# High and low planes in one stationary operand, four projections per head instead of six

## The reference

```python
q_bits = (np.einsum('bhsd,dk->bhsk', q, proj) > 0)      # 6 bits, same for k
mask = q_bucket[:, :, :, None] == k_bucket[:, :, None, :]
scores = np.where(mask, scale * q @ k.T, -1e9)
attn = softmax(scores)                                   # sum + 1e-9
x = attn @ v                                             # 2 batches, 8 heads, 768 positions, 64 wide
x = elu(x @ w_in) @ w_out                                # 1536 tokens, 512 -> 2048 -> 512
out = (s * relu(x @ w2_in)**2 + b) @ w2_out
```

## Time and profile before

| | us |
|---|---|
| median of 3 runs | 739.97 (739.96 to 742.11) |
| profiled execution | 740.75 |
| its span, first to last instruction | 738.9 |
| PE busy | 729.4 (99%) |
| DVE busy | 558.3 (76%) |
| ACT busy | 502.0 (68%) |
| POOL busy | 497.3 (67%) |

### The profile page before, as it was taken

The page is one execution under the profiler, slowest core; times in us unless marked ns, Lnnn a source line. Parts: engine busy times, 40 slices in busy tenths (PEclk is TensorE's granted clock), DMA queues, the critical chain, the costliest instruction groups (busy, mean ns, idle before and its releaser), DMA issues.

```text
span 738.9 us, 14169 instructions
## 1 busy us (share of the span) xinstructions
PE 729.4 (99%) x4617; PEld 666.1 (90%) x4617; DVE 558.3 (76%) x1185; ACT 502.0 (68%) x941; POOL 497.3 (67%) x436
## 2 busy tenths in 40 slices
PE   8999999999999999999999999999999999999998
PEld 5999999999999799989998999889988999899986
DVE  6888888888887887877666777677767776766664
ACT  7888888888885676576556666587566656474552
POOL 6678999999996787835554677676655454744340
PEclk9999999999999999999999999999999999999999
DMA  5676665575514222321122123122112211121101
GB/s 168 156 179 136 165 162 140 156 176 121 138 51 107 68 96 95 114 59 56 31 58 59 58 87 115 58 88 84 58 58 68 80 54 58 58 96 48 58 1 57
DMA packets 78287, 67.82 MB, mean 92 GB/s; under 512 B 9284, under 2 KB 66964, under 8 KB 78228
## 3 DMA queue, kind: packets, MB, share of 16 engines
q1 hardware_dynamic: 77940, 66.80, 33.3%
q10 hardware_dynamic: 288, 0.26, 0.1%
HBM read 46.23 MB, written 3.19 MB: 67 GB/s over the span
## 4 chain that ended last, share of the span: by engine, by line
PE 82%; POOL 7%; issue 3%; DMA 2%; ACT 2%; DVE 2%; SPq 1%; POOLq 0%; DVEq 0%; ACTq 0%
PE acc L928 35%; PE h_ps L908 32%; PE pt_ps L851 5%; PE pv_ps L866 2%; PE pv_ps L867 2%; PE s_ps L837 2%; PE s_ps L838 2%; POOL pt_lo L554 1%; POOL pt_hi L552 1%; DMA qqk<-qqk 1%; DMA qqk<-bits 1%; POOL x L570 1%; POOL qqk L542 1%; POOL x_sum L561 1%; POOL xb_lo L680 1%
## 5 line engine op out<-in xcount | busy, mean ns | idle before, releaser
L616 POOL TENSOR_TENSOR wi_lo<-w_raw,wi_hi 128x512 fp32r<-128x512 f32 x96 | 100.0, 1043 | 186.8 <-ACT wi_hi L1022 185.3
L908 PE MATMUL h_ps<-xb_hi,wi_hi 128*128 128x256 f32 x672 | 190.6, 284 | 1.8 <-DVE h_ps L1372 1.0
L908 PE MATMUL h_ps<-xb_hi,wi_lo 128*128 128x256 f32 x672 | 190.1, 283 | 0.0
L908 PE MATMUL h_ps<-xb_lo,wi_hi 128*128 128x256 f32 x672 | 190.1, 283 | 0.0
L908 PEld LDWEIGHTS h_ps<-xb_hi,wi_hi 128*128 128x128 f32 x672 | 128.7, 192 | 5.2 <-DVE h_ps L1372 2.3
L908 PEld LDWEIGHTS h_ps<-xb_lo,wi_hi 128*128 128x128 f32 x672 | 128.8, 192 | 1.8
L908 PEld LDWEIGHTS h_ps<-xb_hi,wi_lo 128*128 128x128 f32 x672 | 128.8, 192 | 0.0
L621 POOL TENSOR_TENSOR wi_lo<-wi_sum,wi_hi 128x512 fp32r<-128x512 f32 x96 | 123.1, 1308 | 1.5 <-ACT wi_hi L1022 1.5
L1144 ACT ACTIVATE r_sb<-h_sb 128x512 f32<-128x512 f32 x96 | 60.0, 625 | 76.7 <-DVE h_sb L1361 76.7
L1199 DVE TENSOR_SCALAR_CACHE_REDUCE probs<-s_ps 128x768 f32<-128x768 f32 x96 | 91.8, 957 | 10.8 <-PE s_ps L838 7.9
L928 PE MATMUL acc<-g_hi,wo_late 128*128 128x512 f32 x288 | 91.8, 390 | 0.0
(11 more groups left out here) (118 smaller groups left out, 1676.4 us busy)
## 6 DMA issues: line engine op xcount, KB each, us to landing
w_raw<-w_in_dram SPq DMA_DIRECT2D x96, 256.0 KB, 3.1
wo_raw<-w_out_dram SPq DMA_DIRECT2D x32, 256.0 KB, 2.9
raw<-qk_dram SPq DMA_DIRECT2D x15, 384.0 KB, 6.0
qqk<-kt SPq DMA_DIRECT2D x15, 384.0 KB, 4.5
raw_v<-v_dram SPq DMA_DIRECT2D x16, 192.0 KB, 4.8
x_parts<-x_second SPq DMA_DIRECT2D x16, 192.0 KB, 6.4
qqk<-qqk SPq DMA_DIRECT2D x15, 192.0 KB, 2.7
kt<-kt SPq DMA_DIRECT2D x15, 192.0 KB, 4.6
```

The source lines that it names most:

```text
L616: return nc.gpsimd.tensor_tensor(flat(lo[:, j]), w_raw[step % 2][:, cols], flat(hi[:, j]).bitcast(F32), ALU.subtract)
L908: last = mm(h_ps[bank][:, 0:Q], w[i][:, k * P:(k + 1) * P], x[j][:, k * Q:(k + 1) * Q], start=k == 0 and m == 0, stop=k == DK - 1 and m == 2)
```

## The change

`planes_hi` and `planes_lo` become one tensor `planes_parts`, 112 columns for each half: 48 high, 16 zero, 48 low. A matmul with all 112 columns as the stationary operand gives high by `kt1` in rows 0 to 47 and low by `kt1` in rows 64 to 111 of `prep_ps`, so that a head has four matmuls: one such for each half, and two of the high part by `kt2`. The two parts have to be added: ACT copies rows 64 to 111 into `z_low` (`keep_low`, in unit 0 of each head, behind its two copies of transposes), DVE adds rows 0 to 47 to it in place, waits for that, and makes the bits from it. The bits move from unit 0 of a head to unit 1 (`BITS_UNIT` = 1). For head 1, in the first pair, they stay at the end of unit 0. POOL zeroes the 16 columns once.

```diff
--- before.py
+++ after.py
@@ -49,7 +49,7 @@
 SETS = ROUND = 3
 
 
-SIGN_UNIT, BITS_UNIT, ROUND_UNIT = TILES - 1, 0, 0
+SIGN_UNIT, BITS_UNIT, ROUND_UNIT = TILES - 1, 1, 0
 
 FIRST_LATER = 1
 WARM_GAP = 2
@@ -77,6 +77,9 @@
 
 BIT_PAIR = 2 * BITS
 SIGN_ROWS = 4 * BIT_PAIR
+
+LOW_ROW = 64
+PLANE_ROWS = LOW_ROW + SIGN_ROWS
 HEAD_ROWS = BIT_ROWS + BIT_PAIR
 
 
@@ -179,8 +182,9 @@
         planes_in_sb = sb("planes_in_sb", [P, C_END], F32, att)
         planes0 = sb("planes0", [P, 2, BIT_ROWS], F32, att)
         planes = sb("planes", [P, 2, BIT_PAIR, 2, 2], F32, att)
-        planes_hi = sb("planes_hi", [P, 2 * SIGN_ROWS], F32R, att)
-        planes_lo = sb("planes_lo", [P, 2 * SIGN_ROWS], F32R, att)
+
+        planes_parts = sb("planes_parts", [P, 2, PLANE_ROWS], F32R, att)
+        z_low = sb("z_low", [SIGN_ROWS, HALF], F32, att)
         ones = sb("ones", [P, HT], F32, att)
         v_nat = [sb(f"v_nat{n}", [P, TILES, 2 * DH], F32R, att) for n in range(2)]
 
@@ -287,6 +291,8 @@
         wo_hi_done = sem("wo_hi_done")
         wo_split = sem("wo_split")
         z_done = sem("z_done")
+        z_low_kept = sem("z_low_kept")
+        z_added = sem("z_added")
         bits_done = sem("bits_done")
         bits_copied = sem("bits_copied")
         inv_out = [sem(f"inv_out{n}") for n in range(2)]
@@ -751,8 +757,9 @@
             nc.gpsimd.memset(ones[:], 1.0).then_inc(ones_ready, 1)
             nc.gpsimd.memset(planes[:], 0.0).then_inc(planes_cleared, 1)
             nc.gpsimd.memset(planes0[:], 0.0).then_inc(planes_cleared, 1)
+            nc.gpsimd.memset(planes_parts[:, :, SIGN_ROWS:LOW_ROW].bitcast(F32), 0.0).then_inc(planes_cleared, 1)
             pool.wait_ge(ones_ready, 1)
-            pool.wait_ge(planes_cleared, 2)
+            pool.wait_ge(planes_cleared, 3)
             for n, cols in enumerate(halves):
                 pool.wait_ge(rows0_in[n], 16)
                 if n == 1:
@@ -812,13 +819,13 @@
                 pe.wait_ge(planes_split, 1)
                 pe.wait_ge(qk_split, head)
                 wait(pe, bits_done, head - 1)
-                dst = prep_ps[0:SIGN_ROWS, 0:HALF]
-                for n in range(2):
-                    cols, plane = slice(n * HALF, (n + 1) * HALF), slice(n * SIGN_ROWS, (n + 1) * SIGN_ROWS)
-                    mm(dst, planes_hi[:, plane], kt1[buf][:, cols], start=n == 0, stop=False)
-                    mm(dst, planes_lo[:, plane], kt1[buf][:, cols], start=False, stop=False)
-                    last = mm(dst, planes_hi[:, plane], kt2[buf][:, cols], start=False, stop=n == 1)
-                last.then_inc(z_done, 1)
+                high = prep_ps[0:SIGN_ROWS, 0:HALF]
+                both = prep_ps[0:PLANE_ROWS, 0:HALF]
+                first, second = [kt1[buf][:, cols] for cols in halves]
+                mm(both, planes_parts[:, 0, :], first, start=True, stop=False)
+                for n, cols in enumerate(halves):
+                    mm(high, planes_parts[:, n, 0:SIGN_ROWS], kt2[buf][:, cols], start=False, stop=False)
+                mm(both, planes_parts[:, 1, :], second, start=False, stop=True).then_inc(z_done, 1)
 
             def keep_warm(count, zeros):
                 for _ in range(count):
@@ -1047,6 +1054,12 @@
                 wait(act, scores_done, TILES * (head - SETS + 1))
                 copy(kt1[buf][:], raw[par][:]).then_inc(qk_hi, 1)
 
+            def keep_low(head):
+
+                act.wait_ge(z_done, head)
+                wait(act, bits_done, head - 1)
+                copy(z_low[:], prep_ps[LOW_ROW:PLANE_ROWS, 0:HALF]).then_inc(z_low_kept, 1)
+
             def unit(i, k, place, more=True):
                 u, t = UNITS * i + k, k % TILES
 
@@ -1060,6 +1073,8 @@
                     exp(u + 1, (k + 1) % UNITS)
                 split_hi(i, u, k, 0)
                 split_hi(i, u, k, 1)
+                if t == 0 and (k < TILES or more):
+                    keep_low(2 * i + k // TILES + 1)
                 if first and k == 1:
                     round_qk(2, 0, 2, 1)
 
@@ -1067,7 +1082,7 @@
             act.wait_ge(ones_ready, 1)
             nc.scalar.activation(row_sum[:, 0, 0:1], ones[:, 0:1], ACT.Exp)
             act.wait_ge(planes_built, 3)
-            copy(planes_hi[:], planes[:].rearrange("p n r w m -> p (n r w m)")).then_inc(planes_rounded, 1)
+            copy(planes_parts[:, :, 0:SIGN_ROWS], planes[:].rearrange("p n r w m -> p n (r w m)")).then_inc(planes_rounded, 1)
             act.wait_ge(rows0_in[0], 16)
             copy(kt1[0][top, halves[0]], raw[0][top, halves[0]]).then_inc(k0_hi, 1)
             copy(qt1[0][top, halves[0]], raw[0][low, halves[0]]).then_inc(q0_hi, 1)
@@ -1188,9 +1203,11 @@
 
             def write_bits(head):
                 rows = slice(0, SIGN_ROWS)
-                dve.wait_ge(z_done, head)
+                dve.wait_ge(z_low_kept, head)
+                tt(z_low[:], prep_ps[rows, 0:HALF], z_low[:], ALU.add).then_inc(z_added, 1)
                 wait(dve, bits_copied, 16 * head - 16)
-                to_bits(bits[:], prep_ps[rows, 0:HALF], rows, C_THR, C_AMP).then_inc(bits_done, 1)
+                dve.wait_ge(z_added, head)
+                to_bits(bits[:], z_low[:], rows, C_THR, C_AMP).then_inc(bits_done, 1)
 
             def keep_scores(u, k):
 
@@ -1230,7 +1247,7 @@
                 u, third, t = UNITS * i + k, k % HT, k % TILES
                 first = isinstance(i, int) and i == 0
 
-                if t == BITS_UNIT and (k < TILES or more) and not (first and k == 0):
+                if t == BITS_UNIT and (k < TILES or more) and not (first and k < TILES):
                     write_bits(2 * i + k // TILES + 1)
                 if third == 1 and not (first and k < 2 * HT):
                     keep_x(i, k // HT - 2)
@@ -1247,14 +1264,14 @@
             nc.vector.memset(pt_hi[0][:, 0, :].bitcast(F32), 0.0).then_inc(zeros_ready, 1)
             nc.vector.memset(row_sum[:, :, 1:2], EPS).then_inc(eps_ready, 1)
             dve.wait_ge(planes_landed, 16)
-            dve.wait_ge(planes_cleared, 2)
+            dve.wait_ge(planes_cleared, 3)
             laid, sign = [planes_in_sb[:, c:c + 2 * BIT_PAIR].rearrange("p (w r) -> p w r", w=2) for c in (C_PROJ, C_SIGN)]
             tt(planes0[:, :, 0:BIT_PAIR], laid, sign, ALU.mult).then_inc(planes_built, 1)
             for n in range(2):
                 tt(planes[:, n, :, :, n].rearrange("p r w -> p w r"), laid, sign, ALU.mult).then_inc(planes_built, 1)
             dve.wait_ge(planes_rounded, 1)
-            tt(planes_lo[:], planes[:].rearrange("p n r w m -> p (n r w m)"), planes_hi[:].bitcast(F32),
-               ALU.subtract).then_inc(planes_split, 1)
+            tt(planes_parts[:, :, LOW_ROW:PLANE_ROWS], planes[:].rearrange("p n r w m -> p n (r w m)"),
+               planes_parts[:, :, 0:SIGN_ROWS].bitcast(F32), ALU.subtract).then_inc(planes_split, 1)
             dve.wait_ge(k0_hi, 1)
             tt(kt2[0][top, halves[0]], raw[0][top, halves[0]], kt1[0][top, halves[0]].bitcast(F32),
                ALU.subtract).then_inc(k0_lo[0], 1)
```

## The result

| | before | after |
|---|---|---|
| median of the runs | 740.01 us (739.96 to 742.11, 4 runs) | 766.93 us (764.11 to 767.52, 4 runs) |
| the profiled run | 740.75 us, span 738.9 | 764.11 us, span 762.0 |
| ratio after / before | | 1.035 (1.033 to 1.037) |

The change makes the kernel 26.9 us slower by the medians. The prediction was slower too, but by half of that: 753.5, with 759 as the far end. The profiled run of the changed kernel is its quickest one; between the two profiled spans lie 23.1 us, and the terms further down are measured in these.

What follows compares the result with a forecast made beforehand. PE was taken to bound the attention stage, almost without waits. Terms +13.4 (heads 2 to 15), +1.0 (head 1) and -0.6 (DMA of bits) sum to +13.8 us; forecast 753.5 us, range 747 to 759.

Steps and rivals of the forecast that it cites:

- The mechanism: Attention stage: copy, addition and bits delay keep_x in DVE's queue, so PE stops at the pt-by-v product; nothing takes it back.
- the price of the bits instruction: DVE, start of unit 1: bits from SBUF priced by the row from PSUM, 0.669 us, 0.54 to 0.73 with the step.
- stops at the product, heads 2 to 15: PE waits for keep_x at the product of pt and v, about 1.2 us; 1.31 us a head taken.
- T: Start of the first transposes of a head, the zero for its times; PE wanted the pv product at T + 2.64.
- two matmuls fewer: PE, each head: two of six projections removed, 2 x 0.173 = 0.35 us gained.
- head 1: Its bits stay in unit 0; signs, copy and addition make the splits later, +1.0 us, no gain.
- DMA of bits: PE's one wait of 0.6 us for this transfer was taken as gone, -0.6, with 0 as the other end.
- A: Rival: DVE's added work stays covered in the attention stage, POOL limits the gain; 4.0 us faster, 736 us; 9%.
- the margin of 0.44 us: Unit 1, before the change: keep_x ended at T + 2.20, PE wanted the pv product at T + 2.64.
- B: The forecast case: DVE's queue stalls PE in each head; alone 749 to 757 us; 75%.
- C: Rival: as B, and the DMA of bits becomes late too; some four heads with 1 us stalls, 758 us; 12%.
- D: Rival: stalls and gain about cancel through some missed slack; 740 us; 4%.

Runs made afterwards that it cites:

- four products alone: Changed kernel without ACT's copy and DVE's addition, bits made from the high rows alone and in unit 0: 742.55 us, 1.004 of before.
- the first experiment: Changed kernel with DVE's sum written back into PSUM and the bits made from there: 756.52 us, 1.022 of before.
- the last experiment: Changed kernel with POOL's subtraction of 768 columns written as two of 384: 759.04 us, 1.025 of before.
- the first two: Changed kernel with the sum kept in PSUM, 756.52 us; and changed kernel with z_low in SBUF as three blocks of 128 columns, 130 apart, 756.66 us.
- the comparison: Changed kernel; ACT's copy negated and ahead of its transposes' copies, DVE only compares, ACT scales to bits in unit 1, w_raw1 loaded in pair 5: 751.40 us.
- the bits one unit later: Kernel before, six products, with only the bits moved from unit 0 to the start of unit 1: 743.28 us, 1.005 of before.
- the early copy: The first experiment's kernel with ACT's copy of the low part ahead of its two copies of transposes in unit 0: 744.84 us, 1.005 of before.

## Why the prediction was right in sign and half the size

**The mechanism held.** PE's stop, where it stands, for whom, in how many heads, and that nothing takes it back: all as forecast. So did the gain per head (0.35 us, by four products alone), the hidden weight load, ACT's copy (0.49), the addition (0.55), and the missing cost of the place of the bits on DVE. The first experiment is the sum put to the test: from before to it the last transposes of the attention stage move by 13.8 us (224.95 to 238.76), and the sum was 13.8. That it agrees to the tenth is in part luck: the stops are right within 0.3 us, and three smaller terms, each off by 0.4 to 0.9 us, cancel (last column of the table below).

**The step that failed** is the price of the bits instruction: "I take the same instruction's row", 0.669 us, "0.54 to 0.73 with the step". The new instruction reads SBUF, and that row is of one that reads PSUM. It took 0.47 to 2.04 us, 1.13 in the mean. The forecast did see that its speed would differ, and put a faster one on the side of a smaller loss; it did not ask what the faster form has to wait for.

What the runs show of it: the fast form doesn't run beside POOL, but for a short overlap. In 13 of the 15 heads the bits end 0.20 to 0.22 us behind the end of a POOL instruction that began before them or, in heads 2, 4, 14 and 15, up to 0.06 us after they did (ends in head 1: 16.00 and 16.21; head 3: 48.53 and 48.74; head 10: 152.84 and 153.05; head 14: 212.20 and 212.41). Only in heads 6 and 8, where POOL's instruction ends within 0.17 us of their start, do they take their 0.47. The two kernels whose bits have the slower form ran them past the same POOL work in 0.66 to 0.67 us each time. POOL was busy for 13.29 of 13.53 us, so nearly every bits instruction meets one. It waits for as much as is left of it or, where that one ends within 0.1 us of its start (heads 4 and 15), for the next. That the wait is for POOL's running instruction is shown by the last experiment, that it belongs to the fast form alone by the first two.

The Trainium skill has the rule, in "SBUF — State Buffer", section "SBUF: two separate sides": VectorE and GpSimd share one pair of ports, and it is an exclusive lock held for a whole instruction, wanted by a VectorE operation in a two-port mode or by any GpSimd one, and got by the one that starts first. The trace agrees on the waiting, with the 0.20 us above as the time from the end of the one to the end of the other, but not on who is first: in four heads the bits begin ahead of POOL's by the profile and wait all the same. The ports themselves no run here shows. "VectorE: DVE Perf Modes", section "The perf-mode tier table", from which the forecast took the double rate, is borne out where POOL leaves room: the forecast's estimate was 0.2 us off each instruction, and 0.47 us stands against 0.66. But by that the forecast had 751 us, and the kernel took 767: the price of the fast form stands on the other page, on which the forecast did not draw.

**The terms, by the profiled spans.** Forecast +13.8; measured +23.1 for the changed kernel and, up to the last transposes, +13.8 for the first experiment.

| | forecast | measured | first experiment |
|---|---|---|---|
| stops at the product, heads 2 to 15 | 14 x 1.31 = 18.3 | 24.2 (start of the product less T + 2.64, summed) | 18.6 |
| two matmuls fewer | 14 x -0.35 = -4.9 | -4.9 | -4.9 |
| head 1 | +1.0 | +2.7 (T of head 1 is 0.35 early, T of head 2 2.30 late) | +0.6 |
| DMA of bits | -0.6 | -0.6 | +0.3 (a wait of 0.9 where before has 0.6) |
| rest, the clock after the stops of heads 2 and 3 in it | 0 | +1.7 (what is left) | -0.7 (what is left) |

The stops alone are 5.9 of the missing 9.3 us; their spread is 1.13 to 2.62 us, and the seven shortest are below 1.55, near the forecast. Head 1 is 1.7 more: its bits took 1.93 us, and the clock fell behind its stop. The rest is 1.7 more: the clock took 1.19 us in each of heads 2 and 3 by the distances above, and against this stand some 0.7 us of small losses that the kernel before has among its own heads and that show alone in the first experiment, where no clock falls in this stage. So the lengthened bits and the half clock behind their stops account for the whole distance between the profiled runs. The difference between the medians, 26.9 us, is larger than between these two runs; the other runs of the changed kernel have no trace, so which heads were worse in them stays open. That its waits depend on how two queues fall against each other, and that its runs spread over 3.4 us, goes with it.

**The rivals.** A, the cover holds, is out: the margin of 0.44 us was what it seemed. B is what came, at a higher price. C is out for this kernel: no wait for the DMA of bits is left. It describes a part of most of the others, from 0.9 us in the first to 9.3 in the comparison. D is out with a distance of 26.9 us. One limit of A deserves a line: had the cover held, the gain would still not have come, as four products alone show. The forecast put the limit at POOL. PE's waits there are for the DMA of bits, and the chain behind them runs through POOL and through SP's queue; no run tells the two apart.

**The feed-forward stage** was taken as untouched. That holds for the changed kernel (23.1 us at the last transposes, 23.1 at the end). In the first two experiments it cost 2.1 and 2.3 us more: one wait for the first u_sb of 2.0 us, where the kernel before has one of 0.6, and half clock for a while after (PEclk 0.96 from 255 to 300 us). With it, 13.8 + 2.1 = 15.9 us is the distance of the first experiment's span, 754.8, from before. Why the entry into the stage falls so late there and not in the changed kernel was not tried.

## What to carry to other kernels

An instruction's price belongs to its operands' memory and layout, not to its name: when an operand moves from PSUM to SBUF, look for a row with that form, and where there is none, let the range hold the longest instruction that the neighbour engine runs. A faster form of VectorE beside a full GpSimd can be the slower choice; a source in PSUM (0.669 us) or one in blocks (0.664) kept the time constant, and shortening the GpSimd instruction shortened the wait.

A gain of matmuls is real only if the transfers and the other engines behind it have the same margin; a single short wait for a DMA in the trace before is a warning, and so is a chain that runs through another engine than the one that looks full.

## What the runs showed that was not expected

- A VectorE instruction on fp32 from SBUF to SBUF, 48 x 384, took 0.47 us where GpSimd's running instruction ended within 0.17 us of its start, and 1.91 to 2.04 us beside one of 1.8 us that began with it; the next GpSimd one was longer as well (1.94 us in head 3, where the same line took 1.81 in head 1).
- The same instruction from three blocks of 128 columns, 130 apart, took 0.664 us, waited for nobody, and cost the kernel 10 us less.
- In the changed kernel the stops of PE of heads 1, 2 and 3 (3.05, 2.37 and 2.37 us of idle time) were followed by half clock; that of head 5 (2.37 as well) and all shorter ones were not. The length alone doesn't decide it: with the bits one unit later a wait of 1.67 us was followed by half clock, and with the early copy one of 2.15 was not. What does decide it was not tried.
